# Router embedding projected unscaled, its norms applied to the logits; last tile in banks of its own; token products ahead of two roundings

## The chip, the cores and the metric

The kernel runs on 1 core of one Trainium2 chip. The metric is the device time of one launch in microseconds (us). Before the change, three runs took 866.5 us (median), 865.98 us and 868.57 us. A separate execution under the hardware profiler took 874.52 us; its span from the first to the last instruction is 872.7 us. All profile times below are counted from the start of that span.

The engines are PE (TensorE, matrix products into PSUM), DVE (VectorE), ACT (ScalarE), POOL (GpSimd) and SP (SyncE, which issues most DMA transfers). Each engine works through its own list of instructions in order and waits on semaphores that the others raise.

## The reference

Three steps follow one another, all in float32:

```
# 1. gated linear attention: 4 batches x 8 heads, 768 steps, head size 48
state = alpha[t] * state + outer(k[t], v[t]);   y[t] = q[t] @ state
# 2. mixture of experts on x = y as [3072 tokens, 384], 8 experts, one expert per token
xn = x / (norm(x) + 1e-6);   en = emb / (norm(emb) + 1e-6)
logits = xn @ en.T / tau;    idx = argmax(logits)
gate = softmax(logits)[idx]  (sum + 1e-9)
out[idx == e] = gate * (relu(x @ w1[e]) @ w2[e])      # w1 384x1024, w2 1024x384
# 3. a dense layer: h = out @ w_in (384x2048); g = max(0.01 h, h); result = g @ w_out
```

The divisor `norm(emb) + 1e-6` is one number per expert, and tau is one number. So the division of the logits may stand before or behind the product with x.

## The kernel before, in words

**Attention.** Time is cut into 6 chunks of 128 steps, times 4 batches: 24 tiles, numbered 0 to 23 (`num(c, b)`; tile 23 is chunk 5, batch 3). The chunk loop is written out for the first and last chunk, and a hardware loop does the middle ones. Within a chunk the recurrence is turned into matrix products: DVE `prepare` builds running products of alpha by two scans (L808, L816); POOL `prepare` scales q and k with them (`qt` L526, `kt` L531); PE `scores` multiplies them (L1164) and transposes kt (L1170); DVE `mask` (L824) applies the causal mask; PE `values` (L1199), `from_state` (L1207) and `outer` (L1219) make the result and the state; DVE `advance` (L841, L843) and POOL `scale_state` (L539) carry the state on. The engines are staggered by hand: in its step for a tile, DVE prepares the tile two ahead and masks the tile one ahead, then advances its own; PE does the scores of the tile one ahead, then `turn_and_project` of the tile one behind, then `values`, `outer` and `from_state` of its own. Nothing else sets the order.

**Rows and logits.** The result of a tile comes out transposed, in two PSUM banks (`yps`, the banks 4 and 5 of `twin`). ACT `copy_yT` (L627) copies it to SBUF (`xTs`). `turn_and_project` (L1179) multiplies it with `turn`, a matrix that holds an identity (it turns the result back into rows of x) and, beside it, the transposed embedding (it makes the logits), into bank 7. ACT `copy_x` then copies the logits (L635) and the rows (L636) out of bank 7 and squares and sums the rows (L639) for the norm of x. SP stores the rows to DRAM (L391).

**Embedding before.** SP loads the embedding `embs` and `taus` (L410, L411) behind the first tiles' loads. ACT sums its squares (L647) and takes a root (L649, with the load of an ACT table). DVE `scale_emb` (L847 to L854, six operations chained by semaphores and a reciprocal of tau) scales the embedding by the inverse norm; PE `turn_emb` (L1229) transposes it; DVE `place_emb` (L858) puts it into `turn`. `turn_and_project` of tile 0 waits for that (`turn_ready`).

**Routing.** After the last tile DVE works through a long chain on [128 tokens, 24 tiles, 8 experts] (L905 to L1007): maximum, winner, rank, position in a list sorted by expert. ACT takes the root of the row norms (L669), the exponential (L671), and rounds the six pieces of expert 0's weights (L352, `split_hi`; DVE `split_lo`, L358, makes the remainders). POOL and ACT multiply window masks (`win_hot`, L1004) with gates (L559, L678) and token numbers (L676). PE sums them by slot (L1263: tokens, L1273: gates) against `slot_hot` (L1007). DVE turns the sums into index tables (L1014 to L1024), and POOL gathers the token rows by indirect DMA (L573). Then the windows of 128 slots run: PE L1282/L1289 transpose, L1302 first product, L1313 transpose, L1322 second product.

**Fillers.** `keep_busy` (L1155) issues matmuls whose result nobody reads, in counts set by hand (line 277). Each of these 128x128 float32 products shows as two matmul records in the trace.

**The dense layer** (L1372, L1379) follows over 6 groups of 512 tokens; the diff does not touch it.

Of the kernel before, what the change touches and what calls it, by code (L numbers as in the profile page):

```python
# [16 lines left out]
F32 = mybir.dt.float32  # L17
# [7 lines left out]
def build(nc, qka, v, emb, tau, w1, w2, w_in, w_out, x_dram, y_dram, out):  # L25
# [35 lines left out]
    with ExitStack() as ctx:  # L61
# [6 lines left out]
        low = [ctx.enter_context(nc.psum_tensor(f"bank{i}", [P, 512], F32)) for i in range(4)]  # L68
# [16 lines left out]
        with ExitStack() as phase:  # L85
# [22 lines left out]
            embn = sb("embn", [E, 4])  # L108
            turn = sb("turn", [P, PAIRS, PW + E])
# [37 lines left out]
        seeds = bank[3][:, :].rearrange("p (a t) -> p a t", t=L)  # L147

        yps = twin[:, :, 0:2 * L]
        knps = bank[6][:, 0:PAIRS * PW]  # L150
        rowps = bank[7]
        rows_in = rowps[:, :].rearrange("p (a r d) -> p a r d", a=PAIRS, r=PAR)[:, :, :, 0:HD]
        lgps = rowps[:, :].rearrange("p (a x) -> p x a", a=PAIRS)[:, PW:PW + E, :]
        prefps, totps = bank[0][:, 0:E * TILES], bank[1][:, 0:E * TILES]
        tokps, gateps, idleps = bank[2][:, 0:WC], bank[3][:, 0:2 * WC], bank[6][:, 0:P]
# [40 lines left out]
        turn_ready = sem("turn_ready")  # L196
        alpha_in = [sem(f"alpha_in{j}") for j in range(BATCHES)]
# [79 lines left out]
        START_BUSY, HOT_BUSY, POS_BUSY, SLOT_BUSY, GATE_BUSY, GATHER_BUSY, Y_BUSY = 12, 12, 27, 3, 2, 3, 26  # L277
# [16 lines left out]
        def is_first(c):  # L294
            return isinstance(c, int) and c == 0

# [69 lines left out]
        def _(sp):  # L366
# [43 lines left out]
            sp.dma_start(embs[:, :], emb).then_inc(emb_in, 16)  # L410
            sp.dma_start(taus[:, :], tau.to_broadcast([P, 1])).then_inc(emb_in, 16)  # L411
# [191 lines left out]
        def _(act):  # L603
# [19 lines left out]
            def copy_yT(c, b):  # L623
                n = num(c, b)
                act.wait_ge(y_ready, n + 1)
                wait_from(act, turned, n - 1)
                act.activation(xTs[0:PW, b % 2].rearrange("p (s n) -> p s n", s=2), yps[0:PW], ACT.Copy).then_inc(xT_ready, 1)  # L627

            def copy_x(c, b):
# [5 lines left out]
                act.activation(lgq[:, ds(n * E, E)], lgps, ACT.Copy).then_inc(lg_copied, 1)  # L635
                act.activation(xs[:, b].rearrange("p (a r d) -> p a r d", a=PAIRS, r=PAR), rows_in, ACT.Copy).then_inc(x_ready, 1)  # L636
# [3 lines left out]

            seed(0, 0)
# [3 lines left out]
            seed(0, 1)  # L645
            act.wait_ge(emb_in, 32)
            act.activation(squares[0:E, :], embs[:, :], ACT.Square, accum_out=embn[:, 0:1]).then_inc(emb_squared, 1)  # L647
            act.wait_ge(emb_squared, 1)
# [5 lines left out]
            def step(c, b):  # L654
# [6 lines left out]
                if within(before[0]):  # L661
                    copy_x(*before)
# [808 lines left out]
```

## Time and profile before

| what | value |
|---|---|
| three timed runs | 866.5 us median (865.98 to 868.57) |
| profiled execution | 874.52 us, span 872.7 us |
| PE busy | 848.6 us, 97% of the span |
| DVE / ACT / POOL busy | 417.9 / 342.8 / 160.2 us |
| mean granted TensorE clock | 0.982 of full speed |

Stages of the span: attention from 0 to about 124.5 us, routing from there to about 154.8 us, the windows to about 454 us, the dense layer to the end.

How to read it: a busy PE is not PE at its peak, since matmuls are pipelined and fillers count as busy. The share of a whole span says little about a stage of 20 us; what matters there is which wait ends last, and at which clock PE ran.

### The profile page before, as it was taken

How to read it: one execution, taken by the hardware profiler on the slowest of the kernel's cores; microseconds unless marked ns; L12 is line 12 of the kernel's file. 1: busy time of each engine (PE TensorE's matmuls, PEld its weight loads, DVE VectorE, ACT ScalarE, POOL GpSimd, SP SyncE). 2: the span in 40 equal slices, each digit the busy share in tenths (PEclk: the TensorE clock that was granted, in tenths of full speed). 3: DMA queues.
4: the chain of work that ended last, by engine and by line, in shares of the span. 5: the costliest groups of instructions: out<-in, count | busy, mean ns of one | idle time of the engine just before them, and what ended most of it. 6: DMA issues, size and time to landing. Idle time of an engine off the chain costs nothing.

```text
span 872.7 us, 17335 instructions
## 1 busy us (share of the span) xinstructions
PE 848.6 (97%) x5556; PEld 765.2 (88%) x5557; DVE 417.9 (48%) x640; ACT 342.8 (39%) x662; POOL 160.2 (18%) x210
## 2 busy tenths in 40 slices
PE   6999989999999999999997999999999999999998
PEld 5888879899999889999985999998999998999897
DVE  7899956645445444545254443443343343343332
ACT  3455545444444344445243333333333333333323
POOL 5566614222232232222120000000000000000000
PEclk9899996999999999999998999999999999999999
DMA  9999760542355152354105001101100200100101
GB/s 224 210 220 220 181 200 20 191 170 102 112 191 182 30 189 88 128 184 150 60 1 109 1 1 50 24 1 34 38 0 7 65 0 0 37 1 1 37 1 36
DMA packets 45266, 76.25 MB, mean 87 GB/s; under 512 B 16231, under 2 KB 35731, under 8 KB 45232
## 3 DMA queue, kind: packets, MB, share of 16 engines
q1 hardware_dynamic: 41264, 64.98, 26.8%
q0 software_dynamic: 3968, 10.82, 3.6%
q8 instruction: 21, 0.34, 0.2%
q14 instruction: 13, 0.11, 0.0%
HBM read 61.63 MB, written 15.53 MB: 88 GB/s over the span
## 4 chain that ended last, share of the span: by engine, by line
PE 93%; DVE 2%; DMA 1%; issue 1%; ACT 1%; SPq 1%; POOL 0%; POOLq 0%; DVEq 0%
PE bank L1372 23%; PE bank L1379 23%; PE bank L1322 15%; PE bank L1302 15%; PE bank L1313 3%; PE bank L1199 3%; PE bank L1179 3%; PE bank L1164 2%; PE bank L1207 1%; PE bank L1289 1%; PE bank L1155 1%; PE bank L1170 1%; PE bank L1219 1%; DMA taus<-tau 1%; PE bank L1273 1%
## 5 line engine op out<-in xcount | busy, mean ns | idle before, releaser
L1372 PE MATMUL bank<-yT,wts 128*128 128x512 f32 x864 | 217.2, 396 | 6.3 <-DVE yT L1113 6.3
L1379 PE MATMUL bank<-wts,gs 128*128 128x384 f32 x1152 | 217.3, 337 | 0.0
L1379 PEld LDWEIGHTS bank<-wts,gs 128*128 128x128 f32 x1152 | 204.5, 188 | 8.9 <-issue 0.4
L1372 PEld LDWEIGHTS bank<-yT,wts 128*128 128x128 f32 x864 | 162.0, 189 | 36.8 <-DVE yT L1113 7.2
L1131 DVE TENSOR_TENSOR g<-bank,small 128x512 f32<-128x512 f32 x96 | 66.5, 693 | 180.4 <-ACT small L763 180.4
L1302 PE MATMUL bank<-wts,gxT 128*128 (+1 forms) x558 | 142.0, 399 | 0.4 <-DVE gxT L1053 0.4
L1322 PE MATMUL bank<-wts,hT 128*128 x744 | 137.3, 339 | 1.5 <-DVE hT L1084 1.5
L763 ACT ACTIVATE small<-bank 128x512 f32<-128x512 f32 x96 | 57.5, 599 | 190.9 <-PE bank L1372 190.8
L1322 PEld LDWEIGHTS bank<-wts,hT 128*128 128x128 f32 x744 | 128.4, 188 | 1.9 <-issue 1.8
L1302 PEld LDWEIGHTS bank<-wts,gxT 128*128 128x128 f32 x558 | 102.3, 189 | 19.9 <-issue 0.8
L1133 DVE TENSOR_TENSOR gs<-g,gs 128x512 fp32r<-128x512 f32 x96 | 66.6, 693 | 67.1 <-ACT gs L766 67.1
L766 ACT ACTIVATE gs<-g 128x512 fp32r<-128x512 f32 x96 | 60.7, 633 | 72.9 <-DVE g L1131 72.9
L710 ACT ACTIVATE hT<-bank 128x512 fp32r<-128x512 f32 x62 | 33.7, 597 | 126.6 <-PE bank L1313 126.6
L358 DVE TENSOR_TENSOR wts<-raw,wts 128x1024 f32 (+1 forms) x60 | 70.0, 1220 | 18.7 <-ACT wts L352 18.7
L595 POOL DMA_INDIRECT y_rows<-ys,idst x31 | 32.2, 1040 | 197.3 <-DVE ys L1096 197.3
L1084 DVE TENSOR_TENSOR hT<-bank,hT 128x512 fp32r<-128x512 f32 x62 | 40.0, 686 | 51.4 <-ACT hT L710 51.4
L352 ACT ACTIVATE wts<-raw 128x1024 f32 (+1 forms) x60 | 59.0, 1058 | 2.5 <-PE bank L1322 2.5
L1096 DVE TENSOR_SCALAR ys<-bank,slot_gate 128x384 f32<-128x384 f32 x31 | 19.1, 615 | 47.4 <-PE bank L1322 47.4
L686 ACT ACTIVATE hs<-bank 128x512 f32<-128x512 f32 x62 | 37.2, 599 | 5.3 <-PE bank L1302 5.3
L1045 DVE TENSOR_TENSOR gxT<-bank,gxT 128x384 fp32r<-128x384 f32 x30 | 16.7, 558 | 43.5 <-ACT gxT L682 43.5
L573 POOL DMA_INDIRECT xg<-x_rows,isrc x28 | 30.6, 1092 | 25.2 <-POOL isrc L568 25.2
L526 POOL TENSOR_TENSOR qt<-qkas,decay 112x512 f32<-112x512 f32 x24 | 30.7, 1280 | 16.8 <-DVE decay L808 16.8
(163 smaller groups left out, 716.8 us busy)
## 6 DMA issues: line engine op xcount, KB each, us to landing
raw<-w SPq DMA_DIRECT2D x14, 1536.0 KB, 7.1
qkas<-qka SPq DMA_DIRECT2D x40, 289.5 KB, 5.0
vs<-v SPq DMA_DIRECT2D x24, 192.0 KB, 4.7
x_rows<-xs SPq DMA_DIRECT2D x24, 192.0 KB, 4.2
yl<-y_rows SPq DMA_DIRECT2D x24, 192.0 KB, 4.5
out<-os SPq DMA_DIRECT2D x5, 768.0 KB, 4.3
raw<-w_in SPq DMA_DIRECT2D x2, 1536.0 KB, 6.8
raw<-w_out SPq DMA_DIRECT2D x2, 1536.0 KB, 6.7
```

What stands on the lines that cost most here:

```text
L352: act.activation(set_of(par, 0, cols), raw[:, cols], ACT.Copy).then_inc(w_hi, 1)
L358: dve.tensor_tensor(set_of(par, 1, cols), raw[:, cols], set_of(par, 0, cols).bitcast(F32), ALU.subtract).then_inc(w_lo, 1)
L686: act.activation(hs[:, u, half * HALF:(half + 1) * HALF], hps[u][half][:, :], ACT.Relu).then_inc(relu_done, 1)
L763: act.activation(small[:, f % 2], gps[f % 2][:, :], ACT.Copy, scale=0.01).then_inc(small_done, 1)
L766: act.activation(gs[:, f % 4, 0], g[:, f % 2], ACT.Copy).then_inc(g_hi, 1)
L1084: dve.tensor_tensor(hT[:, 1, h], htps[half][:, :], hT[:, 0, h].bitcast(F32), ALU.subtract).then_inc(ht_lo, 1)
L1131: dve.tensor_tensor(g[:, f % 2], gps[f % 2][:, :], small[:, f % 2], ALU.max).then_inc(g_done, 1)
L1133: dve.tensor_tensor(gs[:, f % 4, 1], g[:, f % 2], gs[:, f % 4, 0].bitcast(F32), ALU.subtract).then_inc(g_lo, 1)
L1302: m = pe.matmul(hps[u][half][:, :], gxT[:, u, x_part, k * P:(k + 1) * P], set_of(par, w_part, slice(n, n + HALF)), start=(k == 0 and (x_pa ...
L1322: m = pe.matmul(yeps, hT[:, h_part, k * P:(k + 1) * P], set_of(par, w_part, slice(n, n + D)), start=(k == 0 and (h_part, w_part) == (0, 0) ...
L1372: m = pe.matmul(gps[f % 2][:, :], wts[:, 0, w_part, n:n + P], yT[:, u, y_part, k], start=(k == 0 and (w_part, y_part) == (0, 0)), stop=(k ...
L1379: m = pe.matmul(ops[tt], gs[:, f % 4, g_part, tt * P:(tt + 1) * P], wts[:, 1, w_part, f * D:(f + 1) * D], start=(f == 0 and (g_part, w_par ...
```

## The change: what it does

1. ACT issues the loads of the embedding and tau as its first two instructions, instead of SP behind the first loads. ACT squares the embedding ahead of the seed of tile 1.
2. PE transposes the unscaled embedding after the first 12 fillers, and 5 more fillers (`FILL_BUSY`) follow before the scores of tile 0. ACT, not DVE, copies the transposed embedding into `turn`, ahead of its root. After the products of tile 0, PE waits for `turn` and issues 5 more fillers.
3. DVE computes the inverse norms in the last chunk's first step (`norm_emb`), as a diagonal matrix `embd` of 8 x 8. PE spreads it over all 128 partitions by one small product with ones (`spread_norms`), DVE multiplies it with 1/tau (`keep_norms`), and the logits are multiplied with that, in place of the multiplication with 1/tau alone.
4. For tile 23, the result goes to banks 2 and 3 (`twin_low`), its rows to bank 6. PE does `values` and `from_state` of tile 23 ahead of `turn_and_project` of tile 22. ACT squares the rows of tiles 22 and 23 after copying those of tile 23.
5. ACT rounds four pieces of expert 0's weights, then does the 24 token products and the 12 gate remainders, then the last two pieces. PE's wait for all six pieces ahead of the gate sums becomes a wait for the first.
6. `HOT_BUSY` is 13 instead of 12; the idle fillers write bank 4 instead of 6.

```diff
+        yps = [twin[:, :, 0:2 * L], twin_low[:, :, 0:2 * L]]
+        rowps = [bank[7], bank[6]]
+        embps, normps = bank[7][:, 0:PAIRS * E], bank[2][:, 2 * L:2 * L + E]
...
-        START_BUSY, HOT_BUSY, ... = 12, 12, ...
+        START_BUSY, FILL_BUSY, HOT_BUSY, ... = 12, 5, 13, ...
+        def is_final(c, b):
+            return int(is_last(c) and b == BATCHES - 1)
...  SP
-            sp.dma_start(embs[:, :], emb).then_inc(emb_in, 16)
-            sp.dma_start(taus[:, :], tau.to_broadcast([P, 1])).then_inc(emb_in, 16)
...  ACT
+            act.dma_start(embs[:, :], emb).then_inc(emb_in, 16)
+            act.dma_start(taus[:, :], tau.to_broadcast([P, 1])).then_inc(emb_in, 16)
             seed(0, 0)
             ... (identity into turn)
-            seed(0, 1)
             act.wait_ge(emb_in, 32)
             act.activation(squares[0:E, :], embs[:, :], ACT.Square, accum_out=embn[:, 0:1]).then_inc(emb_squared, 1)
+            seed(0, 1)
+            act.wait_ge(emb_turned, 1)
+            act.activation(turn[0:PW, :, PW:PW + E], embps[0:PW]..., ACT.Copy).then_inc(turn_ready, 1)
             act.wait_ge(emb_squared, 1)
             act.activation(embn[:, 1:2], embn[:, 0:1], ACT.Sqrt).then_inc(root_done, 1)
...
                 copy_yT(c, b)
                 if within(before[0]):
-                    copy_x(*before)
+                    copy_row(*before)
+                    if not is_final(c, b):
+                        square_row(*before)
-            copy_x(CH - 1, BATCHES - 1)
+            copy_row(CH - 1, BATCHES - 1)
+            for b in (BATCHES - 2, BATCHES - 1):
+                square_row(CH - 1, b)
...
-            split_hi(act, 0, 0, range(PIECES))
+            split_hi(act, 0, 0, range(4))
             for c in range(TILES): ... token products
             for c in range(LO_TILES, TILES): ... gate remainders
+            split_hi(act, 0, 0, range(4, PIECES))
...  DVE
-                dve.tensor_scalar(embs[:, :], embs[:, :], embn[:, 3:4], None, ALU.mult).then_inc(emb_scaled, 1)
+                dve.tensor_scalar(embd[:, :], ident[0:E, 0:E], embn[:, 3:4], None, ALU.mult).then_inc(emb_scaled, 1)
                 link(dve.reciprocal(rtau[:, :], taus[:, :]))
-            def place_emb(): ...
+            def keep_norms():
+                dve.wait_ge(norms_spread, 1)
+                dve.tensor_scalar(embr[:, :], normps, rtau[:, 0:1], None, ALU.mult).then_inc(norms_kept, 1)
...
                 if within(two[0]):
                     prepare(*two)
-                if is_first(c) and b == 1:
-                    place_emb()
                 if within(one[0]):
                     mask(*one)
-                if is_first(c) and b == 0:
-                    scale_emb()
+                if is_last(c) and b == 0:
+                    norm_emb()
+                if is_last(c) and b == 2:
+                    keep_norms()
...
-            start("main", dve.tensor_scalar(flat(lg[:, :, :]), lgs[:, :], rtau[:, 0:1], None, ALU.mult))
+            dve.wait_ge(norms_kept, 1)
+            start("main", dve.tensor_tensor(lg[:, :, :], lgs[:, :]..., embr[:, :].unsqueeze(1).to_broadcast([P, TILES, E]), ALU.mult))
...  PE
             def values(c, b):
-                wait_from(pe, xT_ready, n)
+                if is_final(c, b):
+                    pe.wait_ge(norms_kept, 1)
+                else:
+                    wait_from(pe, xT_ready, n)
+            def spread_norms():
+                pe.wait_ge(emb_scaled, 1)
+                pe.wait_ge(state_tmp, num(CH - 1, 0))
+                pe.matmul(normps, ones[0:E, :], embd[:, :], start=True, stop=True).then_inc(norms_spread, 1)
             keep_busy(START_BUSY, bank[0][:, 0:P], ones[:, :], ones[:, :])
+            turn_emb()
+            keep_busy(FILL_BUSY, bank[0][:, 0:P], ones[:, :], ones[:, :])
             scores(0, 0)
             def step(c, b):
                 if within(after[0]):
                     scores(*after)
-                if within(before[0]):
+                if within(before[0]) and not is_final(c, b):
                     turn_and_project(*before)
                 values(c, b)
+                if is_last(c) and b == 1:
+                    spread_norms()
                 ... (outer, from_state)
                 if is_first(c) and b == 0:
-                    turn_emb()
+                    pe.wait_ge(turn_ready, 2)
+                    keep_busy(FILL_BUSY, bank[7][:, 0:P], ones[:, :], ones[:, :])
+                if is_final(c, b):
+                    turn_and_project(*before)
...
-            pe.wait_ge(w_hi, PIECES)
+            pe.wait_ge(w_hi, 1)
```

## Rows read from the trace of the kernel before

**Rows 1.** Page, part 4: the chain that ended last, by engine.

```profile
PE 93%; DVE 2%; DMA 1%; issue 1%; ACT 1%; SPq 1%; POOL 0%; POOLq 0%; DVEq 0%
```

**Rows 2.** PE by windows: stretch, us, busy (records), granted clock, DMA share, GB/s.

```profile
18.00:20.00 2.00, 0.94 (x12) 0.85 1.12 187
...
26.00:28.00 2.00, 2.00 (x22) 0.95 1.09 200
...
138.00:139.00 1.00, 1.00 (x10) 0.93 0.00 0
...
155.00:156.00 1.00, 1.00 (x3) 0.54 1.02 414
```

**Rows 3.** Timeline of the first tiles: start, duration, instruction, idle before and releaser.

```profile
2.97 5.49 PE L1155 MATMUL bank<-ones 128*128 128x128 f32 x24 [2.97 <-POOL prio L515]
...
4.52 0.36 SPq L411 DMA_DIRECT2D taus<-tau  x1
...
8.39 1.51 PE L1164 MATMUL bank<-qt,kt 48*128 48x128 f32 x16
...
9.42 0.58 ACT L647 ACTIVATE squares<-embs 8x448 f32<-8x448 f32 x1 [2.42 <-DMA taus<-tau]
...
10.02 1.29 DVE L824 TENSOR_TENSOR probs<-bank,causal 128x512 f32<-128x512 f32 x2 [0.29 <-PE bank L1164]
...
11.69 1.22 DVE L808 TENSOR_TENSOR_SCAN decay<-qkas,bank 112x512 f32<-112x512 f32 x1 [0.39 <-ACT bank L615]
...
15.48 0.13 DVE L847 TENSOR_SCALAR embn<-embn 8x1 f32<-8x1 f32 x1
...
16.44 0.44 DVE L853 TENSOR_SCALAR embs<-embs,embn 8x448 f32<-8x448 f32 x1
...
16.80 0.14 DVE L854 RECIPROCAL rtau<-taus 128x1 f32<-128x1 f32 x1
...
20.17 2.03 PE L1179 MATMUL bank<-turn,xTs 112*128 112x120 f32 x8 [1.23 <-DVE turn L858]
...
24.77 0.36 DVE L841 COPY state_sum<-bank 112x192 f32<-112x192 f32 x1 [3.55 <-PE bank L1219]
```

**Rows 4.** Timeline of the last chunk of the attention.

```profile
109.94 1.21 DVE L808 TENSOR_TENSOR_SCAN decay<-qkas,bank 112x512 f32<-112x512 f32 x1
...
112.71 1.28 POOL L531 TENSOR_TENSOR kt<-qkas,inv 112x512 f32<-112x512 f32 x1 [0.20 <-DVE inv L816]
...
114.23 1.16 PE L1164 MATMUL bank<-qt,kt 48*128 48x128 f32 x16
...
119.49 1.12 PE L1179 MATMUL bank<-turn,xTs 112*128 112x120 f32 x8 [1.23 <-ACT xTs L627]
...
122.27 0.60 ACT L627 ACTIVATE xTs<-bank 112x512 f32<-112x512 f32 x1 [2.24 <-PE bank L1207]
...
125.21 0.52 ACT L639 ACTIVATE squares<-xs 128x384 f32<-128x384 f32 x1
...
126.11 0.18 DVE L910 TENSOR_SCALAR nrm<-nrm 128x24 f32<-128x24 f32 x1 [0.26 <-ACT nrm L669]
```

**Rows 5.** Timeline of the routing, up to the first window's product.

```profile
129.96 5.78 ACT L352 ACTIVATE wts<-raw 128x1024 fp32r<-128x1024 f32 x6
...
133.71 0.56 DVE L1004 TENSOR_TENSOR decay<-count,posf 128x384 f32<-128x384 f32 x1
...
135.64 5.18 ACT L676 ACTIVATE wts<-decay,token 128x32 fp32r<-128x32 f32 x24
...
136.31 1.15 PE L1263 MATMUL bank<-wts 128*128 128x32 f32 x6 [0.84 <-DVE wts L1007]
...
137.02 2.44 DVE L1007 TENSOR_TENSOR wts<-count,posf 128x768 fp32r<-128x768 f32 x2
...
143.79 0.19 DVE L1014 COPY slot_val<-bank 128x31 f32<-128x31 f32 x1 [3.69 <-PE bank L1263]
...
154.82 1.44 PE L1302 MATMUL bank<-wts,gxT 128*128 128x512 f32 x3 [0.43 <-DVE gxT L1053]
```

More of the change, by code:

```diff
@@ L66, in keep @@
             return ctx.enter_context(nc.sbuf_tensor(name, shape, dt))
-        low = [ctx.enter_context(nc.psum_tensor(f"bank{i}", [P, 512], F32)) for i in range(4)]
+        low = [ctx.enter_context(nc.psum_tensor(f"bank{i}", [P, 512], F32)) for i in range(2)]
+        twin_low = ctx.enter_context(nc.psum_tensor("bank23", [P, 2, 512], F32))
+        low += [twin_low[:, 0, :], twin_low[:, 1, :]]
         twin = ctx.enter_context(nc.psum_tensor("bank45", [P, 2, 512], F32))
@@ L626, in copy_yT, with copy_row @@
                 wait_from(act, turned, n - 1)
-                act.activation(xTs[0:PW, b % 2].rearrange("p (s n) -> p s n", s=2), yps[0:PW], ACT.Copy).then_inc(xT_ready, 1)
-            def copy_x(c, b):
+                act.activation(xTs[0:PW, b % 2].rearrange("p (s n) -> p s n", s=2), yps[is_final(c, b)][0:PW],
+                               ACT.Copy).then_inc(xT_ready, 1)
+            def copy_row(c, b):
                 n = num(c, b)
@@ L644, in _ @@
                            ACT.Copy).then_inc(turn_ready, 1)
-            seed(0, 1)
             act.wait_ge(emb_in, 32)
             act.activation(squares[0:E, :], embs[:, :], ACT.Square, accum_out=embn[:, 0:1]).then_inc(emb_squared, 1)
+            seed(0, 1)
+            act.wait_ge(emb_turned, 1)
+            act.activation(turn[0:PW, :, PW:PW + E], embps[0:PW].rearrange("p (a e) -> p a e", a=PAIRS),
+                           ACT.Copy).then_inc(turn_ready, 1)
             act.wait_ge(emb_squared, 1)
@@ L1175, in turn_and_project, with result @@
                 pe.wait_ge(xT_ready, n + 1)
-                wait_from(pe, x_ready, n)
+                if not is_final(c, b):
+                    wait_from(pe, x_ready, n)
                 pe.wait_ge(turn_ready, 2)
+                rows = rowps[is_final(c, b)]
                 for a in range(PAIRS):
-                    m = pe.matmul(rowps[:, a * L:a * L + PW + E], xTs[0:PW, b % 2, a * L:(a + 1) * L], turn[0:PW, a, :],
+                    m = pe.matmul(rows[:, a * L:a * L + PW + E], xTs[0:PW, b % 2, a * L:(a + 1) * L], turn[0:PW, a, :],
                                   start=True, stop=True)
                 m.then_inc(turned, 1)
-            def result(a, r):
+            def result(c, b, a, r):
                 at = a // 2 * L
-                return yps[head_rows(r ^ (a & 1)), a % 2, at:at + L]
+                return yps[is_final(c, b)][head_rows(r ^ (a & 1)), a % 2, at:at + L]
             def values(c, b):
@@ L1198, in values @@
                         h = a * PAR + r
-                        m = pe.matmul(result(a, r), vs[:, b, h * HD:(h + 1) * HD],
+                        m = pe.matmul(result(c, b, a, r), vs[:, b, h * HD:(h + 1) * HD],
                                       probs[:, b % 2, r, a, :], start=(a < 2), stop=is_first(c), skip_group_check=True)
@@ L1206, in from_state @@
                     for r in range(PAR):
-                        m = pe.matmul(result(a, r), state[head_rows(r), b, a, :],
+                        m = pe.matmul(result(c, b, a, r), state[head_rows(r), b, a, :],
                                       qt[head_rows(r), b, a, :], start=False, stop=True, skip_group_check=True)
```

47 lines of the change are left out of this document (25 added, 22 removed).

## Prediction, made before the changed kernel ran

> **What bounds the kernel now.** I read the page's chain first: PE holds 93% of it [rows 1], so an edit on another engine pays only where PE waits, or where PE is slow. The granted clock by windows comes second. It shows full speed (2.4 GHz) nearly everywhere and two long stretches at half speed (1.2 GHz) near this change [rows 2]: one from about 19.4 us to 26.2 us, the other from 138.9 us to 155.9 us (a slice at 0.85 spent 30% of its 2 us at half speed). Around the first fall, PE was busy only 0.94 of 2 us. Third come the timelines of the three places that the diff touches.
>
> In the first tiles the reader is to see a chain through the embedding. The load of tau is issued at 4.52 us, ACT squares at 9.42 us after waiting 2.42 us for it, DVE spends 15.48 to 16.94 us on the scaling, PE idles until `turn` is placed, and starts the turn of tile 0 at 20.17 us [rows 3]. By then its clock has fallen: those 8 records take 2.03 us, against 1.12 us for 8 at full speed [rows 4]. DVE pays: its advance of tile 1 waits 3.55 us for PE and starts at 24.77 us [rows 3].
>
> At the end of the attention PE waits 1.23 us for ACT's copy of each of the last two results, and the routing's chain then waits for the root of the row norms until 126.11 us [rows 4]. In the routing, PE starts its slot sums at 136.31 us, although DVE's first marks come earlier: ACT's token products start only at 135.64 us, behind six roundings of 0.96 us each (5.78 us in all) [rows 5].
>
> The stretch at half speed in the routing belongs to the profiled execution. That took 874.5 us, 8.0 us above the median of 866.5 us. At most half of the 17.0 us at half speed, 8.5 us, can come from it, and most of it was PE-bound. So I take the 8.0 us as its price, and take it that the timed runs went without it. The first stretch I take for the rule in the timed runs too, since PE is idle there in every execution that waits for `turn` in this way.
>
> **The change part by part.**
>
> *Start, against.* After 12 fillers (24 records in 5.49 us, 0.229 us each, half of that at full speed [rows 3]) PE now does four tiny transposes, about 0.4 us, and 5 more fillers, 10 records. All at half speed they are 2.3 us, all at full 1.15 us. The scores of tile 0 at 8.39 us run 1.51 us against 1.16 us later [rows 3, 4], so the clock rose while they ran; I take 1.4 us. The scores then start near 10.15 us instead of 8.39 us, their mask on DVE ends near 12.6 us instead of 11.3 us, and DVE's preparation of tile 2 starts 0.9 us late (11.69 us before [rows 3]). The bounds of this step are 0.7 and 1.9 us late.
>
> *Start, for.* DVE loses the scaling: 15.48 to 16.94 us, 1.46 us [rows 3]. A preparation is 2.65 us (from 109.94 us to just before POOL's next product at 112.71 us, which waits 0.20 us for it [rows 4]) and a mask 1.29 us [rows 3]. So its advance of tile 0 comes at 12.6 + 2.65 + 1.25 = 16.5 us instead of 16.98 us, the preparation of tile 3 at 16.8 us, the mask of tile 2 ends at 20.7 us. PE meanwhile does the scores of tile 1 from 12.7 us (1.16 us, and about half of that for the transposes behind them), values and outer (about 1.4 us) to 15.8 us, the 5 new fillers (1.2 us) to 17.0 us, scores of tile 2 to 18.7 us, and turn, values and outer in 2.3 us (half of the 4.6 us from 20.17 to 24.77 us, since PE has no idle stretch that would bring the clock down) to 21.1 us. The advance of tile 1 then starts at 21.15 us instead of 24.77 us: 3.6 us earlier. All that follows up to the last chunk hangs on this chain and shifts with it. If the clock falls as before, the gain is about 1.3 us; if also the scores of tile 0 come at the late bound, nothing is left. The upper bound is 4.2 us, with the scores of tile 3 no longer at half speed either.
>
> The two loads move from SP's queue to ACT's. SP's later loads are issued some 0.8 us earlier (two issues of about 0.4 us), which nobody waits for. ACT issues before its first seed, which waits for alpha anyway. A load on ACT's queue this early is not in the trace; the one on SP's took 4.9 us from issue (4.52 to 9.42 us [rows 3]). Issued near 1.7 us it would be there by 6.6 us; PE asks for it at about 8.2 us, so it costs nothing, with 1.6 us of cover. *The Trainium skill ("DMA: Bandwidth & Descriptors", section "Issuing engines are not separate DMA queues") says that transfers issued by different engines run on the same 16 DMA engines and interleave, so that another issuer saves only the time of issuing. By that rule the load does not get faster on ACT's queue, which speaks against the edit; no row of before tests it. It is the mechanism of the third rival.* ACT's copy of the embedding into `turn` (a few tenths) and its root lie ahead of the seed of tile 2, which DVE now wants only at 12.6 us; before it waited 0.39 us for that seed.
>
> *Last chunk, against.* The norm chain moves to DVE right behind the mask of tile 21, where DVE has no gap: at 109.94 us it goes straight on to prepare tile 23, POOL makes kt at 112.71 us, PE the scores of tile 23 at 114.23 us [rows 4]. The six operations and the reciprocal cost 1.46 us less 0.3 us for the smaller last product (0.44 us against 0.13 us for the smallest [rows 3]), with links about 1.25 us. POOL's kt and the scores of tile 23 wait behind it; PE idles that long. The bounds are 0 (if the link waits hide) and 1.5 us. The spreading product on PE (two records of at most 0.15 us, as the turn's 1.12 us for 8 [rows 4]) and the DVE operation that follows (0.13 us) lie in front of values of tile 23, which comes 1.3 us later.
>
> *Last chunk, for.* PE no longer turns tile 22 before values of tile 23, so the wait of 1.23 us and the turn of about 1.1 us leave the way to the last result: 2.35 us. With the 1.25 us lost, ACT's last copy starts at 121.2 us instead of 122.27 us (1.1 us earlier), and turn and logits follow. But ACT now squares two tiles of rows behind it, 0.65 us each (125.21 us to the root just behind [rows 4]), so the root comes 1.1 − 0.65 = 0.45 us earlier. DVE's chain has that wait in its order, so the winner and all behind it gain 0.45 us. The multiplication by a spread norm instead of a scalar, and one more filler pair, are hundredths or hidden behind that wait. Bounds: 0.2 us (1.5 us lost) to 1.7 us (nothing lost).
>
> *Routing.* Four roundings from 129.5 us end at 133.4 us; the first 12 token products can then start with DVE's window mark at 133.9 us instead of 135.64 us, and the second 12 follow the second mark (before 137.02 us) at 136.7 us. At 0.216 us each (5.18 us for 24 [rows 5]) the last ends at 139.3 us instead of 140.8 us. DVE's last slot marks come at 139.0 us (137.02 + 2.44 − 0.45 [rows 5]); they were late by 139.5 us before and hidden by ACT. So the slot sums end 1.4 us earlier, 0.95 us of it new. What is late next is DVE, hence not more; the bounds are 0.45 and 1.4 us in all. The tables, the gathers and the first product at 154.82 us hang on the slot sums (DVE waits 3.69 us for them at 143.79 us [rows 5]). The last two roundings move to about 142 to 144 us; DVE needs them only after the tables and three remainders, so they cost nothing.
>
> *Sum.* 874.5 − 8.0 (half speed in the routing, not in the timed runs) − 3.6 (start) − 1.4 (end and routing) = 861.5 us, or 5.0 us (0.6%) under the median of the timed runs.
>
> **The rivals.**
> 1. *The start gives little:* the clock falls in the first tiles as before, or was not low in the timed runs. For it: PE still has idle stretches there, and the new fillers delay the scores. Against it: PE's longest gap goes. Time: 866.5 − 1.3 − 1.4 = 863.8 us, up to 865 us with the late bound.
> 2. *Slower, the clock falls in the routing of the timed runs.* Place: the slot sums, whose records are narrow, behind a new idle time of some 1.3 us before the scores of tile 23. For it: the profiled run fell there at 138.9 us although PE had been counted fully busy in that very microsecond [rows 2]. Against it: the 0.84 us of idle time just before those sums [rows 5] goes. Price 8.0 us: 861.5 + 8.0 = 869.5 us. It turns the change to slower from 5.0 us of its price on, that is if the fall comes before some 10 us of the 17 us are over. *By the Trainium skill ("TensorE: Matmul & The Clock Gate", Part 1) half speed is the default state and activity releases it; the two falls here agree.*
> 3. *The embedding lands late,* and PE, in order, holds the scores of tile 0 for it. Each microsecond after 8.2 us is lost whole. With the landing at 9.42 us as now, 862.7 us; it eats the whole gain from 13.2 us on, 11.5 us after the issue. Against that stands the 4.9 us of the row.
> 4. *It does not do what it says:* ACT's, DVE's and PE's waits only change places, and the sum is within a microsecond or two of 866.5 us.
>
> **How the numbers follow.** Forecast 0.56 (859.5 to 863.8 us), rival 1 0.2, rival 2 0.1, rival 3 0.04, rival 4 0.1. 0.3% is 2.6 us, about what a measurement here can tell from no change. Faster, under 863.9 us: nearly all of the forecast, about a third of rival 1 and half of rival 3, 0.63. Slower, over 869.1 us: two thirds of rival 2 and a share of 4 and of the unknown, 0.13. The rest, 0.24, is within. The range is 859.0 us (upper bounds at the start and in the last chunk together) to 867.4 us (rival 4 with a loss of a microsecond), which leaves out rival 2 and little else.
>
> **What would show it.** Right: the advance of tile 1 near 21 us and PE at full clock from 19 to 26 us; scores of tile 0 near 10 us; 1.3 us of idle PE before the scores of tile 23, and one wait for ACT's copy there instead of two; the root 0.45 us earlier than the shift of the first tiles alone would put it; token products starting with the first window mark; slot sums paced by DVE's marks. Wrong: an advance of tile 1 later than 23 us, half speed in the slot sums, PE waiting for the embedding's load, or gains of the first tiles that are gone again by the middle chunks, where loads would then be late.

## The result, and the profile after

The changed kernel takes 863.4 us (median of 14 runs, 861.14 to 866.56); the kernel before took 868.18 us beside it (14 runs, 865.98 to 876.91). The ratio is 0.9942, 95% interval 0.9918 to 0.9966. By the medians it is 4.8 us faster, where the prediction had 5.0 us. The time itself is 1.9 us above the predicted 861.5 us; 1.7 us of that lie in the base, since the prediction counted from a median of three runs, 866.5 us. A second set of 12 runs gave 865.03 us, ratio 0.9935 (0.9904 to 0.9965), but only 2.9 us by the medians (867.94 us before). The ratios also weigh the long runs of before at 874 to 877 us, 2 of 14 in the first set and 5 of 23 in the second; without these the means differ by 3.9 us and 2.8 us.

The profiled execution took 862.47 us, its span is 860.5 us. That is 12.2 us below the profiled execution of before, more than the timed runs give, since that one had its 17 us at half speed in the routing [rows 2]. So the kernel before was profiled again, twice (`before_again`, `before_third`). Both ran the routing at full speed, and they are the measure from here on. Where a time within a profile is given, "before" and "after" mean the first profiles of the two kernels. Starts in us:

| start of | before | before_again | after |
|---|---|---|---|
| scores of tile 0 | 8.39 | 8.34 | 9.86 |
| advance of tile 1 | 24.77 | 24.63 | 20.88 |
| scores of tile 22 | 110.28 | 110.01 | 106.24 |
| ACT's copy of the last result | 122.27 | 121.99 | 116.80 |
| root of the row norms (ACT) | 125.86 | 125.57 | 120.54 |
| slot tokens read (DVE) | 143.79 | 141.23 | 135.24 |
| first window's product | 154.82 | 147.96 | 141.90 |
| profiled time | 874.52 | 866.44 | 862.47 |

Four lines of before_again, for the comparisons further down: the turn of tile 0, the advance of tile 1, the copy of the last logits and the read of the slot tokens.

```profile
20.18 2.03 PE L1179 MATMUL bank<-turn,xTs 112*128 112x120 f32 x8
...
24.63 0.36 DVE L841 COPY state_sum<-bank 112x192 f32<-112x192 f32 x1 [3.41 <-PE bank L1219]
...
124.31 0.20 ACT L635 ACTIVATE lgq<-bank 128x32 f32<-128x32 f32 x1 [0.61 <-PE bank L1179]
...
141.23 0.19 DVE L1014 COPY slot_val<-bank 128x31 f32<-128x31 f32 x1 [1.41 <-PE bank L1263]
```

The timeline of the first tiles, after; the rows answer to [rows 3].

```profile
0.82 0.61 ACTq L656 DMA_DIRECT2D embs<-emb  x1
...
1.47 0.38 ACTq L657 DMA_DIRECT2D taus<-tau  x1
...
5.46 0.57 ACT L663 ACTIVATE squares<-embs 8x448 f32<-8x448 f32 x1 [1.06 <-DMA taus<-tau]
...
9.86 1.16 PE L1190 MATMUL bank<-qt,kt 48*128 48x128 f32 x16
...
15.56 1.38 PE L1181 MATMUL bank<-ones 128*128 128x128 f32 x10
...
18.41 1.06 PE L1207 MATMUL bank<-turn,xTs 112*128 112x120 f32 x8
...
20.43 0.18 ACT L625 ACTIVATE bank<-qkas 112x4 f32<-112x4 f32 x1 [4.17 <-DMA qkas<-qka]
...
20.88 0.36 DVE L866 COPY state_sum<-bank 112x192 f32<-112x192 f32 x1 [0.64 <-PE bank L1250]
```

The turn of tile 0 waits for nothing and takes 1.06 us instead of 2.03 us; DVE's advance of tile 1 waits 0.64 us instead of 3.55 us. PE by windows, after, against [rows 2]: no stretch at half speed at either place.

```profile
18.00:20.00 2.00, 2.00 (x26) 1.00 1.02 194
...
26.00:28.00 2.00, 2.00 (x24) 1.00 0.98 190
...
138.00:139.00 1.00, 1.00 (x10) 1.00 0.00 0
```

The timeline of the last chunk, after, against [rows 4].

```profile
105.90 0.13 DVE L872 TENSOR_SCALAR embn<-embn 8x1 f32<-8x1 f32 x1
...
106.24 1.16 PE L1190 MATMUL bank<-qt,kt 48*128 48x128 f32 x16
...
107.17 1.22 DVE L833 TENSOR_TENSOR_SCAN decay<-qkas,bank 112x512 f32<-112x512 f32 x1
...
111.27 1.16 PE L1190 MATMUL bank<-qt,kt 48*128 48x128 f32 x16 [0.70 <-POOL kt L541]
...
116.64 2.04 PE L1207 MATMUL bank<-turn,xTs 112*128 112x120 f32 x16
116.71 0.19 ACT L654 ACTIVATION_READ_ACCUMULATOR squares<-xs 128x1 f32 x1
116.80 0.58 ACT L637 ACTIVATE xTs<-bank 112x512 f32<-112x512 f32 x1
117.83 0.20 ACT L646 ACTIVATE lgq<-bank 128x32 f32<-128x32 f32 x1 [0.45 <-PE bank L1207]
...
118.72 0.20 ACT L646 ACTIVATE lgq<-bank 128x32 f32<-128x32 f32 x1 [0.32 <-PE bank L1207]
...
120.54 0.22 ACT L693 ACTIVATE nrm<-ss 128x24 f32<-128x24 f32 x1
...
120.79 0.18 DVE L936 TENSOR_SCALAR nrm<-nrm 128x24 f32<-128x24 f32 x1 [0.78 <-ACT nrm L693]
```

The norm chain stands between the mask of tile 21 and the next scan, and PE waits 0.70 us for POOL in front of the scores of tile 23. At the end both turns run as one group of 16 records. The routing, after, against [rows 5]:

```profile
128.39 0.56 DVE L1030 TENSOR_TENSOR decay<-count,posf 128x384 f32<-128x384 f32 x1
...
128.99 2.65 ACT L700 ACTIVATE wts<-decay,token 128x32 fp32r<-128x32 f32 x12 [0.46 <-DVE decay L1030]
...
131.81 2.65 ACT L700 ACTIVATE wts<-decay,token 128x32 fp32r<-128x32 f32 x12 [0.18 <-DVE decay L1030]
...
135.24 0.19 DVE L1040 COPY slot_val<-bank 128x31 f32<-128x31 f32 x1 [0.45 <-PE bank L1307]
```

ACT now waits for each of DVE's window marks, and DVE waits 0.45 us for the slot sums, against 1.41 us in before_again (3.69 us in the first profile of before, which ran this stretch at half speed).

### The profile page after: what moved, and what is told of

Read it like the earlier page. It is cut to its first block, busy times and chain, and to the rows that moved or that the text cites. A ratio compares the mean times of both kernels' runs of the same rounds, so it can differ in the third digit from the quotient of the medians.

```text
span 860.5 us, 17386 instructions
## 1 busy us (share of the span) xinstructions
PE 841.3 (98%) x5580; PEld 758.7 (88%) x5581; DVE 417.7 (49%) x640; ACT 342.9 (40%) x663; POOL 160.3 (19%) x210
## 4 chain that ended last, share of the span: by engine, by line
PE 93%; DVE 3%; DMA 1%; POOL 1%; issue 1%; ACT 0%; SPq 0%; POOLq 0%; DVEq 0%; ACTq 0%
PE bank L1416 24%; PE bank L1423 24%; PE bank L1366 15%; PE bank L1346 15%; PE bank L1357 3%; PE bank L1190 3%; PE bank L1230 2%; PE bank L1207 2%; PE bank L1238 1%; PE bank L1333 1%; PE bank L1196 1%; PE bank L1181 1%; PE bank L1250 1%; DMA yl<-y_rows 1%; POOL kt L541 0%
## 5 line engine op out<-in xcount | busy, mean ns | idle before, releaser
L583 POOL DMA_INDIRECT xg<-x_rows,isrc x28 | 30.6, 1092 | 25.2 <-POOL isrc L578 25.2
```

## The experiments

Ratios are to the kernel before, run in turn on the same chip: e1 to e4 on one, e5 to e8 on another, e9 and the repeats on a third. The kernel before took 867.4 to 867.9 us (median) on these three. All intervals of these runs overlap with that of the changed kernel, so steps of a microsecond or two are read from the traces, and the times tell only whether they fit.

**e1: the new fillers left out.**

```diff
- START_BUSY, FILL_BUSY, ... = 12, 5, ...
+ START_BUSY, FILL_BUSY, ... = 12, 0, ...
```

> The changed kernel without its two groups of 5 new fillers. Theory (the gain of the first tiles comes from PE no longer waiting for the embedding, which alone keeps its clock up): the scores of tile 0 start near 8.9 us instead of 9.86 us, full clock from 16 to 26 us, the advance of tile 1 near 19.5 us instead of 20.88 us; the preparation of tile 4 is then held by its load (its seed waited until 20.43 us for it in the changed kernel), so only about 0.5 us is left at the advance of tile 2 (24.4 us against 24.94 us) and in the total. Rival (the fillers keep the clock up): half speed somewhere between 17 and 27 us, the advance of tile 1 at 22.5 us or later, the total 1.5 to 3 us longer.

Measured: 862.88 us, ratio 0.9922 (0.9885 to 0.9959). The trace's timeline:

```profile
8.72 1.16 PE L1190 MATMUL bank<-qt,kt 48*128 48x128 f32 x16 [0.19 <-POOL kt L541]
...
11.44 2.08 PE L1190 MATMUL bank<-qt,kt 48*128 48x128 f32 x16 [1.02 <-DVE probs L849]
...
21.45 0.36 DVE L866 COPY state_sum<-bank 112x192 f32<-112x192 f32 x1 [0.29 <-PE bank L1250]
```

The clock did fall: the scores of tile 1 took 2.08 us, and PE ran at half speed for 6.8 us, from 11 to 18 us. But the scores of tile 0 came 1.14 us earlier than in after, and the advance of tile 1 only 0.57 us later. So neither expectation held: not full speed and an advance near 19.5 us, and not a loss of 1.5 us or more. In this trace the fillers buy full speed for about what they cost; no gain of theirs can be measured.

**e2: the norm chain late** (`norm_emb` behind the mask of tile 23, the spread in front of the last turns).

```diff
-                if is_last(c) and b == 0:
-                    norm_emb()
                 if is_last(c) and b == 2:
+                    norm_emb()
                     keep_norms()
...
-                if is_last(c) and b == 1:
-                    spread_norms()
                 if is_final(c, b):
+                    spread_norms()
                     turn_and_project(*before)
```

> The changed kernel with the norm chain on DVE behind the mask of tile 23 instead of ahead of the preparation of tile 23, and the spread behind the last result. Theory (the chain costs 1.1 us where it stands, as the scores of tile 23 come 5.03 us after those of tile 22 instead of 3.95 us): scores of tile 23 at 3.95 us behind those of tile 22, PE does not idle 0.70 us there, the root of the norms and all behind it 1.1 us earlier, total 1.1 us shorter. Rival (the way to the last result is set elsewhere, by ACT's copies or DVE's masks): the scores move, the root does not, total within 0.3 us.

Measured: 862.84 us, ratio 0.9933 (0.9898 to 0.9969). In the trace the scores of tiles 22 and 23 stand 3.95 us apart (107.38 and 111.33 us), as in before, against 5.03 us in after: the chain costs 1.08 us there. Only 0.60 us of the 1.1 us expected reaches the root (13.70 us from the scores of tile 22, against 14.30 us). The spread (116.87 us, 0.38 us) now stands in front of the turns, which start behind the last copy instead of ahead of it:

```profile
117.03 0.58 ACT L637 ACTIVATE xTs<-bank 112x512 f32<-112x512 f32 x1
...
117.18 2.04 PE L1206 MATMUL bank<-turn,xTs 112*128 112x120 f32 x16
```

The step is not resolved in the time.

**e3: the last tile in its turn**, as before.

```diff
         def is_final(c, b):
-            return int(is_last(c) and b == BATCHES - 1)
+            return 0
```

> The changed kernel with tile 23 in the same banks as all others, its values behind the turn of tile 22, and each square behind its own copy. Theory (the wait for ACT's copy and the turn, 1.23 + 1.1 us, left the way to the last result): ACT's last copy 2.4 us later, the root, with one square less behind the copy, 2.2 us later, and so the total. Rival (what was gained there was hidden behind the root and the squares): root and total later by 0.5 us at most.

Measured: 864.62 us, ratio 0.9954 (0.9925 to 0.9983). PE's and ACT's timeline:

```profile
120.47 1.12 PE L1205 MATMUL bank<-turn,xTs 112*128 112x120 f32 x8 [1.23 <-ACT xTs L637]
...
123.26 0.60 ACT L637 ACTIVATE xTs<-bank 112x512 f32<-112x512 f32 x1 [2.24 <-PE bank L1233]
124.42 1.12 PE L1205 MATMUL bank<-turn,xTs 112*128 112x120 f32 x8 [1.23 <-ACT xTs L637]
```

Both waits of 1.23 us are back. From the scores of tile 23 to the last copy it takes 7.86 us, in after 5.53 us, in before_again 8.03 us. From the scores of tile 22 to the root it is 16.48 us against 14.30 us: 2.2 us in the trace, as expected. The time points the same way (2.8 us under before by the medians, against 4.8 us), but the intervals overlap.

**e4: all six roundings first**, as before.

```diff
-            split_hi(act, 0, 0, range(4))
+            split_hi(act, 0, 0, range(PIECES))
...
-            split_hi(act, 0, 0, range(4, PIECES))
```

> The changed kernel with all six roundings ahead of the token products. Theory: the token products start near 130.4 us instead of 128.99 us and end near 135.6 us instead of 134.46 us, PE waits before its first slot sums, the slot sums end 1.0 to 1.2 us later and so does the first product (141.90 us in the changed kernel), total 1.0 us longer. Rival (the gathers or DVE's remainders set the first product): slot sums later, first product and total within 0.3 us.

Measured: 863.79 us, ratio 0.9946 (0.9912 to 0.998). Root to the read of the slot tokens: 15.66 us, as in before_again, against 14.70 us in after. The step is worth 0.96 us in the trace; in the time it is not resolved. Lines of this trace; the first two are of its first tiles, have nothing to do with the edit and are needed further down:

```profile
23.30 1.22 DVE L832 TENSOR_TENSOR_SCAN decay<-qkas,bank 112x512 f32<-112x512 f32 x1 [2.00 <-ACT bank L625]
...
24.79 1.69 PE L1206 MATMUL bank<-turn,xTs 112*128 112x120 f32 x8 [0.40 <-issue]
...
139.56 0.19 DVE L1039 COPY slot_val<-bank 128x31 f32<-128x31 f32 x1 [1.40 <-PE bank L1306]
```

**e5: the two loads back on SP**, behind the first tiles' loads.

```diff
-            act.dma_start(embs[:, :], emb).then_inc(emb_in, 16)
-            act.dma_start(taus[:, :], tau.to_broadcast([P, 1])).then_inc(emb_in, 16)
...
             load_v(0, 0)
+            sp.dma_start(embs[:, :], emb).then_inc(emb_in, 16)
+            sp.dma_start(taus[:, :], tau.to_broadcast([P, 1])).then_inc(emb_in, 16)
```

> The changed kernel with the loads of the embedding and tau issued by SP behind the first tiles' loads, as before. In the changed kernel they were there at 5.4 us, 3.6 us after the issue by ACT had ended. Theory (the place in the queue decides): they land near 9.4 us; ACT squares then, so the seed of tile 1 comes near 10.1 us instead of 6.83 us and PE's transposes near 9.4 us instead of 8.23 us; the mask of tile 0 ends near 14.3 us instead of 12.3 us, all behind it and the total 1.9 us later. Rival (the load has cover on either queue): total within 0.3 us.

Measured: 865.31 us, ratio 0.9975 (0.9953 to 0.9997), 2.1 us under before by the medians; more than half of the gain is gone. The timeline:

```profile
9.36 0.58 ACT L663 ACTIVATE squares<-embs 8x448 f32<-8x448 f32 x1 [5.03 <-DMA taus<-tau]
...
9.38 0.38 PE L1257 MATMUL bank<-ident,embs 8*112 8x8 f32 x4 [1.28 <-DMA taus<-tau]
...
10.12 1.22 DVE L833 TENSOR_TENSOR_SCAN decay<-qkas,bank 112x512 f32<-112x512 f32 x1 [3.48 <-ACT bank L627]
...
11.01 1.16 PE L1190 MATMUL bank<-qt,kt 48*128 48x128 f32 x16
```

This is the place of the third rival: PE waits 1.28 us for the embedding, in front of the scores of tile 0. The load holds ACT too. ACT squares the embedding ahead of the seed of tile 1, so DVE's preparation of tile 1 starts at 10.12 us instead of 7.04 us, which the third rival did not count. The clock then fell as well, from 14 to 21 us, and the advance of tile 1 came at 25.72 us. So the early load is a condition of the rest; how much of the loss is the load and how much the clock was not told apart.

**e6: DVE's wait for the root moved behind the winner**, and its five operations on the norms with it.

```diff
-            dve.wait_ge(root_done, 2)
-            start("side", dve.tensor_scalar(safe, root, 1e-30, None, ALU.max))
...
             dve.tensor_tensor(hot[:, :, :], cand[:, :, :], over(best, E), ALU.is_equal).then_inc(hot_ready, 1)
             after("side")
+            dve.wait_ge(root_done, 2)
+            start("side", dve.tensor_scalar(safe, root, 1e-30, None, ALU.max))
```

> The changed kernel with DVE's wait for the root of the row norms, and the operations on it, moved behind the operation that makes the winner. Theory (DVE's main chain waited 0.78 us for a root that it does not need yet): the rank product on PE 0.6 us earlier, the first product and the total 0.5 us shorter. Rival (the operations on the norms now stand in a row behind the winner, and the exponential waits for them): rank product earlier, but the exponential later, and the total within 0.3 us or longer.

Measured: 862.2 us, ratio 0.9932 (0.991 to 0.9953). The timeline:

```profile
120.07 0.22 ACT L693 ACTIVATE nrm<-ss 128x24 f32<-128x24 f32 x1
...
120.76 0.36 DVE L944 TENSOR_TENSOR hot<-cand,red 128x192 f32<-128x192 f32 x1
```

The winner comes 0.69 us behind the root instead of 1.54 us, the exponential 0.25 us later behind the winner; from the scores of tile 22 to the first product 35.10 us instead of 35.66 us.

**e7: the start as before**, with parts 1 to 3 of the change undone (the loads on SP, the transposes behind tile 0, the scaling on DVE) and the rest as changed. The lines are against the changed kernel; those on DVE are left out.

```diff
-            act.dma_start(embs[:, :], emb).then_inc(emb_in, 16)
+            sp.dma_start(embs[:, :], emb).then_inc(emb_in, 16)
...
-            turn_emb()
-            keep_busy(FILL_BUSY, bank[0][:, 0:P], ones[:, :], ones[:, :])
             scores(0, 0)
...
-                    pe.wait_ge(turn_ready, 2)
-                    keep_busy(FILL_BUSY, bank[7][:, 0:P], ones[:, :], ones[:, :])
+                    turn_emb()
```

> The kernel before with the other parts of the change alone: the last tile in banks of its own, the order of roundings and token products, 13 fillers; embedding scaled at the start as before. Theory: first tiles as before (advance of tile 1 near 24.8 us, half speed from about 19 to 26 us), 4.0 us behind the changed kernel; no norm chain in the last chunk, 1.1 us ahead; total 2.9 us above the changed kernel and 2.5 us under the kernel before. Rival (the gain of the first tiles is lost again by the middle chunks, since loads come late): total within 1 us of the changed kernel.

Measured: 864.57 us, ratio 0.9958 (0.9935 to 0.9981). That is 2.9 us under before by the medians, where 2.5 us was expected, but only 1.2 to 1.9 us behind the changed kernel (by the times themselves, or by each one's distance to before), where 2.9 us was expected. The timeline:

```profile
19.79 1.12 PE L1194 MATMUL bank<-turn,xTs 112*128 112x120 f32 x8 [1.24 <-DVE turn L871]
...
22.33 0.36 DVE L854 COPY state_sum<-bank 112x192 f32<-112x192 f32 x1 [1.49 <-PE bank L1235]
```

PE waits for `turn` as in before, but here the clock fell at 11 us and was back at 15 us, so the turn ran at full speed. The advance of tile 1 came at 22.33 us: 1.45 us behind after and 2.30 us ahead of before_again. From the start of the turn to that advance it is 2.54 us here and 4.45 us in before_again, where PE was at half speed: 1.91 us. The other 0.39 us are an earlier start of the turn, since the embedding was there at 9.03 us instead of 9.41 us. So of the 3.75 us between before_again and after, the wait (with a stretch at half speed that cost little) is 1.45 us, and half speed on the turn and the products behind it is 1.91 us, in this one pair of traces.

**e8: e2 and e6 together.** **e9: e8 with the spread behind the turn of tile 23** and 1/tau folded into the diagonal, so that the logits are multiplied with the PSUM bank itself.

```diff
-                    spread_norms()
                     turn_and_project(*before)
...
             turn_and_project(CH - 1, BATCHES - 1)
+            spread_norms()
...
-                dve.tensor_scalar(embd[:, :], ident[0:E, 0:E], embn[:, 3:4], None, ALU.mult).then_inc(emb_scaled, 1)
+                dve.tensor_scalar(embd[:, :], ident[0:E, 0:E], embn[:, 3:4], rtau[0:E, 0:1], ALU.mult, ALU.mult).then_inc(emb_scaled, 1)
```

> The changed kernel with both: norm chain behind the mask of tile 23, and the wait for the root behind the winner. Theory: the two gains add, 1.1 + 0.5 = 1.6 us under the changed kernel, and this beats both kernels. Rival (behind an earlier last copy the root is even later against DVE's chain, so that the two overlap): 1.1 us or less.

> As the version with norm chain and root wait both late, and besides the spreading product on PE behind the turn of tile 23 instead of in front of the turn of tile 22, with 1/tau folded into the diagonal, so that the logits are multiplied straight with the spread norms. Theory (PE has no gap from the scores of tile 23 on, so that the two records of the spread delayed both turns by 0.31 us): from the scores of tile 22 to the first product 34.2 us instead of 34.55 us in that version and 35.66 us in the changed kernel; total 0.3 us under that version. Rival (the spread is now late for the logits): 34.55 us or more.

Measured, e8: 861.94 us, ratio 0.992 (0.9897 to 0.9943), the fastest median of all. From the scores of tile 22 to the first product it takes 34.55 us: 1.11 us less than after, close to the sum of e2's 0.53 us and e6's 0.56 us. The 1.6 us expected did not come, since e2 alone gave half of what it was expected to. e9: 34.21 us, another 0.34 us less as expected, yet the median is 862.76 us (ratio 0.9932, 0.9905 to 0.9959): the step is in the trace, and too small for the time.

**The three repeats.**

> The kernel before unaltered, for a second profile. Theory: PE at half speed somewhere in the first tiles in each execution, the advance of tile 1 between 22.3 us (where the fall ends before the turn of tile 0) and 24.8 us; no half speed in the routing, whose first product then comes 28.5 to 29.0 us behind the root, and the total 866 to 869 us. Rival: half speed in the routing too, total near 875 us.

> The kernel before unaltered, for a third profile; as for the second: half speed in the first tiles, the advance of tile 1 between 22.3 us and 24.8 us, none in the routing.

> The changed kernel unaltered, for its time beside the others and a second profile. Theory (half speed falls at other places from run to run, and costs 3 to 4 us in the attention where it falls): stages without half speed as in the first profile to 0.1 us (5.03 us between the scores of tiles 22 and 23, 35.66 us from the scores of tile 22 to the first product), and some runs near 866 us beside the others near 862.5 us. Rival (the differences between the profiles have another cause): stages differ without half speed in them.

before_again took 866.44 us, before_third 868.12 us. Both fall to half speed at 17 us and stay there to 24 us (6.8 us), and neither does so in the routing. One figure of the expectation was wrong: the first product comes 22.3 to 22.4 us behind the root, not 28.5 to 29.0 us, which was the way at half speed. after_again took 867.42 us, 5 us more than the first profile of the same kernel. Its last chunk and routing are as in after to 0.1 us (5.03 us and 35.70 us), but its first product comes only at 148.12 us, as late as in before_again (147.96 us): the whole gain is gone by then. Its timeline shows where:

```profile
22.19 0.18 ACT L625 ACTIVATE bank<-qkas 112x4 f32<-112x4 f32 x1 [5.72 <-DMA qkas<-qka]
22.40 1.22 DVE L833 TENSOR_TENSOR_SCAN decay<-qkas,bank 112x512 f32<-112x512 f32 x1 [0.95 <-ACT bank L625]
...
40.34 0.60 PE L1190 MATMUL bank<-qt,kt 48*128 48x128 f32 x5
...
42.46 1.49 PE L1190 MATMUL bank<-qt,kt 48*128 48x128 f32 x11 [1.52 <-issue]
...
44.69 1.92 PE L1207 MATMUL bank<-turn,xTs 112*128 112x120 f32 x8
```

Two things show there: the load of tile 4 lands 1.8 us later than in after, and DVE waits 0.95 us for the seed that needs it. And PE stops for 1.52 us in the middle of one group of scores, waiting for nothing that the profile shows; behind the stop the next turn takes 1.92 us, at half speed (42.7 to 49.5 us). The windows there:

```profile
40.00:42.00 2.00, 0.94 (x21) 1.00 1.05 201
42.00:44.00 2.00, 1.54 (x12) 0.67 0.97 230
44.00:46.00 2.00, 2.00 (x11) 0.50 1.12 280
```

## Why the prediction was right, and where a size was off

**The start: right.** Forecast 21.15 us for the advance of tile 1 and 10.15 us for the scores of tile 0; measured 20.88 and 9.86 us. The forecast gain of 3.6 us is 3.75 us against before_again, and the scores of tile 22 still carry 3.77 us of it in after. By its time alone, 863.4 us, the result would fit the first rival (863.8 us) as well; the trace rules that out, since the start gave 3.75 us and not 1.3 us. That the fall of the clock belongs to the timed runs too was right: their mean granted clocks lie mostly at 0.988 to 0.992 before (where they are listed by run) and at 0.992 to 0.996 after. The reason given was half right. The longest gap of PE had to go, and it did, but not by the fillers (e1): turning the embedding early takes away the wait, and the load at the head of ACT's queue lets that happen (e5).

**The embedding's load: right.** From the issue of `taus` to the squares that waited for it passed 4.0 us (1.47 to 5.46 us); behind SP's loads it is 4.8 us (4.52 to 9.36 us in e5). The Trainium skill ("DMA: Bandwidth & Descriptors", section "Issuing engines are not separate DMA queues") holds that another issuer saves only time on the issuing queue. That agrees mostly: of the 3.9 us by which the data came earlier, 3.05 us are the earlier issue; the other 0.85 us are a shorter way from issue to use. Here that was worth taking, though the prediction read the same section as speaking against the edit.

**The last chunk: directions right, one term mis-sized.** The norm chain cost 1.08 us (forecast 1.25 us), and the way from the scores of tile 23 to the last copy became 2.5 us shorter (forecast 2.35 us). The step that failed is the next one, "ACT now squares two tiles of rows behind it, 0.65 us each ..., so the root comes 1.1 − 0.65 = 0.45 us earlier". From the last copy to the root it is 3.74 us against 3.58 us in before_again: 0.16 us more, not 0.65 us. The second square does take 0.71 us (119.18 to 119.89 us), but the prediction left out what happens in front of it. The turn of tile 23 stood directly behind that of tile 22 on PE, 16 records in 2.04 us, so the second logits came 1.92 us behind the copy's start instead of 2.32 us (before_again: 121.99 to 124.31 us), and those 0.40 us paid for most of the 0.56 us by which the rest of the way grew (1.82 us against 1.26 us). The root gained 2.50 − 1.08 − 0.16 = 1.26 us, where the forecast had 0.45 us.

**The routing: right.** 0.95 us forecast, 0.96 us measured from the root to the slot tokens, and undone by e4. The sum for end and routing was 1.4 us and came out as 2.3 us (6.06 us at the first product, less 3.77 us).

**Half speed in the routing: near in its size, wrong in its rule.** It was taken to be 8.0 us and absent from the timed runs. In the first profile of before, root to slot tokens takes 2.27 us longer than in before_again and slot tokens to the first product 4.30 us: 6.6 us, with 1.1 us of half speed still to come. And it is not absent from the timed runs: of before's runs, 2 of 14, 9 of 35, 2 of 31 and 5 of 23 took 874 to 878 us, 6 to 11 us above the median beside them, at mean clocks of 0.977 to 0.982 where these are listed by run (the first profile: 0.982). That it is the routing in each of them was not shown, since a timed run has no trace. None of the 26 runs of after was that long, and none of the 103 of e1 to e9 (870.83 us at most). So the second rival did not happen, and the changed versions do without the long runs. Which part of the change does that stays open: e3, e4 and e7 each undo one and had no such run. The prediction said that the two falls agree with the rule that it cites. The rows do not settle that for the second one: from 135 to 138 us PE was idle 0.87 us in before and 0.86 us in before_again, and only before fell.

**Why 4.8 us and not 6.** To the first product the trace of after gains 6.06 us: 3.77 us at the start, 1.26 us in the last chunk, 1.03 us in the routing. The prediction had 5.0 us there, and let all of it reach the end: "All that follows up to the last chunk hangs on this chain and shifts with it." That step does not hold in every execution. Some of the gain is lost again between 20 and 50 us in some of them.

*Tile 4's load.* ACT's seed of tile 4 waits for it. It comes at 20.43 us in after, at 22.19 us in after_again, 21.91 us in e2, 22.60 us in e9 and 23.09 us in e4. In all but after DVE waits 0.95 to 2.00 us for it. In after_again, e2 and e9 the advance of tile 2 then comes 1.3 to 1.5 us later behind that of tile 1 than in after. In e4 PE is idle as well (1.80 us and 0.40 us), its clock falls at 25.2 us for 3.4 us, and the advance of tile 2 comes 3.9 us later. In before_again the seed comes at 20.05 us, and DVE wants it only behind its advance of tile 1, at 24.63 us. The gain of the first tiles ate that cover of some 4.5 us. "Loads would then be late" stood in the prediction only as a sign of failure, without a price.

*The stop of PE.* 1.52 us, between 40 and 42.5 us, stand in after_again, e3 and e8; 0.26 us in after, 0.15 us in e2, none in the three profiles of before. In the first three PE is then at half speed for 3.4 to 6.8 us, and the way from the advance of tile 2 to the scores of tile 22 takes 84.2 to 86.0 us instead of 80.6 to 81.3 us.

The timed runs agree in part: in the first set after's five runs at 865.9 to 866.6 us have a mean clock of 0.992, the nine at 861.1 to 863.8 us one of 0.994 to 0.996. In the second set the two are less close (865.74 us at 0.995, 863.84 us at 0.992). Which of these stretches made a timed run long was not shown.

*The entry of the dense layer.* Behind the first product the pair of after and before_again parts by chance: 2.1 us of the 6.06 us are gone at the end (3.97 us between the profiled times). There after ran 10.2 us at half speed and before_again 6.8 us. before_third ran 10.2 us too, and there 5.65 us are left. So the end of one pair of profiles does not tell a step of 2 us.

That 4.8 us came out so near to 5.0 us is in part luck. The end and the routing gave 0.9 us more than forecast, and losses that the sum did not hold (in the traces, late loads and stops of PE) took 1.3 us away; in the second set they left 2.9 us.

What remains open is why PE stops there. DMA engines are full at that time (share about 1.0), in after too, where the stop is 0.26 us. In all three long stops one or two packets of an instruction queue (q14) lie inside the stop, and it comes behind the fifth of the 16 records each time. That fits a wait for instructions, but such packets lie in that stretch in both kernels, and no run told these apart.

**A better version.** e8 is ahead of both kernels: 861.94 us, 5.5 us below before by the medians beside it. Against after, its 1.11 us are shown by the trace alone.

## What to carry to other kernels

A wait that lowers TensorE's clock costs twice, and the larger part may be the clock: here 1.45 us of waiting and 1.91 us of half speed. Read the granted clock around a wait before pricing it. When a stage starts earlier, list what it will ask for next and how long that has been lying there: tile 4's load had some 4.5 us of cover and was then late. When two units of work are put directly behind one another, the wait between them goes as well; add up the time to the last result, not the durations one by one. And when a forecast is met, compare it term by term with the trace: here two misses nearly cancelled.

## What was not expected of the hardware

PE can stop for 1.5 us within a group of matmuls that nothing in the profile holds (in three of eleven profiled executions of changed kernels, between 40 and 42.5 us), and stand at half speed behind it. The clock also fell behind little idle time: in e1 PE was busy 0.98 of 2 us (10 to 12 us) when it fell. At the entry of the dense layer every profiled execution of either kernel runs 6.8 to 10.2 us at half speed. The two repeats of before are 0.03 us apart at the first product and 1.7 us in the profiled time, with 6.8 us at half speed in the one and 10.2 us in the other.
